# Attention: where the older head's output is turned, who copies and divides it, and two casts on GpSimd

## The chip, the core and the metric

The kernel runs on one core of one Trainium2 chip. The metric is the device time of one execution in microseconds (us). The core's engines work in parallel and each takes its own instructions strictly in the order in which they are written: TensorE (PE) does the matrix products, VectorE (DVE) and ScalarE (ACT) read and write both SBUF and PSUM here, GpSimd (POOL) works on SBUF, and SyncE (SP) starts most of the transfers. They wait for one another through semaphores.

## What is computed

Attention over 16 heads with queries averaged in pairs, a mixture of 8 experts of which each token takes two, and a last two-layer block. Only the first is touched by the change:

```
q_pool = q.reshape(B, H, S // 2, 2, D).mean(axis=3)         # B=2, H=8, S=1152, D=64
scores = scale * np.matmul(q_pool, k.transpose(0, 1, 3, 2)) # 576 x 1152 per head
scores = scores - np.max(scores, axis=-1, keepdims=True)
attn = np.exp(scores)
attn = attn / (np.sum(attn, axis=-1, keepdims=True) + 1e-09)
x = np.matmul(attn, v)                                      # 576 x 64 per head
logits = x @ w_gate                                         # top 2 of 8 experts per token
```

The inputs are float32, and the kernel keeps that accuracy by splitting operands into a high and a low half.

## The kernel before

**Cycles and heads.** The 16 heads pass through a pipeline of 16 cycles, `cycle(p, hh)` on each engine, of which cycle c = 2p + hh does three things at once. It computes the scores and the products with the values of head c - 1 (numbered from 0, so cycle 1 is head 0), prepares head c (keys and queries transposed, 15 trial score blocks "m" from which the row maxima come), and from cycle 2 on it finishes head c - 2: its output lies as columns in `ot`, is turned back to rows by TensorE (`turn_o`, L1475, which also multiplies with the gate weights), and is divided by the row sums. Cycles 3 to 14 are a hardware loop on PE, ACT and DVE. Cycle 15 prepares the last head, and cycle 16 has no head to prepare and instead computes the routing of the first batch on DVE.

**Steps.** A cycle has 9 steps, one for each block of 128 keys; the text numbers them 1 to 9 (`j` + 1 in the code). In a step PE does the four score matmuls (L1490, L1491) and six value matmuls of an earlier step (L1506 to L1508), ACT takes the exponential twice (`ph` at L788, then in place at L793), and DVE subtracts to get the low half (`low_p`, L1035). PE may start the scores of a step only when the low half of the step two before is done, and the products only when their own low half is done.

**Slots and banks.** Around these, `PLACES` puts up to four smaller jobs in each step: "m" a block for the maximum (PE L1460, reduced by DVE at L1023), "n", "k" and the tail transposes of keys and queries (L1446 to L1451), "q" transposes of the queries' low half with the maxima (L1468), and "o" the turn. They share two PSUM banks in turn (`bank_of`), so a job waits until the one two places before it in the list has been emptied (`bank_free`). Before the change "o" is the last job of step 9, followed by ("k", 3) of the next cycle, four transposes, and then by the scores of step 1. Those scores wait for `qb_ev`, ScalarE's copy of the last "q" piece (L740).

**The output's path before.** After `turn_o`, DVE in `o_out` adds 1e-9 to the five row sums (L1046), takes their reciprocals (L1049), and multiplies 320 output columns (L1061) and 80 gate columns (L1062) out of PSUM. The last of these posts `o_norm`.

**GpSimd** splits the keys, queries and values of the coming head into halves (`split_kq`, `split_v`), copies the keys (`copy_k`), and in its last four heads also splits a quarter of the first expert's weights each (`split_weights`). Heads 2 to 11 are a hardware loop.

**The end of attention.** In cycle 16 PE does one turn ("o" in step 9, head 14), then the products of the last two key blocks, then the turn of head 15, and first-tile and rank products that wait for DVE's routing steps.

## Time and profile before

| | |
|---|---|
| three runs | 854.05, 856.22, 857.81 us (median 856.22) |
| the profiled execution | 854.54 us, of which the trace spans 852.8 us |
| PE busy | 838.9 us, 98% of the span |
| DVE, ACT, POOL busy | 499.0, 422.2, 402.5 us (59%, 50%, 47%) |
| granted TensorE clock | 1.00 over the whole span |

The profile is of one execution. A row of a timeline gives start, duration, engine, line, operation, what is written and read, and how many like it were merged; in brackets stands the idle time ahead of it and who ended it. Matmuls overlap in the pipeline: the duration of one is longer than the distance to the next, so a small stall shows only as a greater distance between two starts, and "busy" hides it. A turn is five matmuls in the program and ten in the trace. Attention ends at about 308 us; the rest of the span is experts and the last block.

### The profile page before, as it was taken

Reading aid. Unit: us, or ns where it says so; the run is one execution under the profiler, and the core shown is the slowest. Engines: PE = TensorE matmul, PEld = TensorE weight load, DVE = VectorE, ACT = ScalarE, POOL = GpSimd, SP = SyncE. Lnnn points to the kernel's source line nnn. Section 1 sums busy time; section 2 is a strip of 40 time slices with the busy share of each in tenths; the row PEclk is TensorE's granted clock in tenths of the full one; section 3 lists DMA queues with packets and bytes.
Section 4 is the critical chain, followed back from the end, with each engine's and each line's share of the span. In section 5 each row is a group of like instructions: output and inputs, shape, how many; then the busy total and the mean of one; then the engine's idle time right before and its main releaser. Section 6 shows DMA issues by size and latency. Waiting matters only on the chain.

```text
span 852.8 us, 15404 instructions
## 1 busy us (share of the span) xinstructions
PE 838.9 (98%) x4868; PEld 744.4 (87%) x4869; DVE 499.0 (59%) x995; ACT 422.2 (50%) x776; POOL 402.5 (47%) x293
## 2 busy tenths in 40 slices
PE   7999999999999999999999999999999999999998
PEld 6899999999999888888887888888888888999997
DVE  7788877888877887322232222222276776676664
ACT  3777777777777763212111211111145665564554
POOL 8554445555877104648959959577532030000000
PEclk9999999999999999999999999999999999999999
DMA  5112211142232015987645545363444020000101
GB/s 146 53 43 62 64 42 42 42 142 67 92 130 102 1 56 181 310 298 241 237 151 172 197 148 184 118 214 115 155 133 152 1 75 27 12 1 0 38 1 38
DMA packets 51521, 91.28 MB, mean 107 GB/s; under 512 B 9376, under 2 KB 18592, under 8 KB 50976
## 3 DMA queue, kind: packets, MB, share of 16 engines
q1 hardware_dynamic: 40832, 67.26, 23.5%
q0 software_dynamic: 3360, 11.01, 4.4%
q10 hardware_dynamic: 7296, 12.59, 4.4%
q8 instruction: 19, 0.31, 0.2%
q14 instruction: 14, 0.11, 0.0%
HBM read 73.78 MB, written 17.06 MB: 107 GB/s over the span
## 4 chain that ended last, share of the span: by engine, by line
PE 89%; DVE 5%; ACT 2%; issue 2%; POOL 2%; DMA 0%; DVEq 0%; POOLq 0%; ACTq 0%
PE ps L1640 10%; PE ps L1642 10%; PE ps L1641 10%; PE ps L1460 5%; PE ps L1490 5%; PE ps L1506 4%; PE ps L1508 4%; PE ps L1507 4%; PE ps L1491 4%; PE ps L1766 4%; PE ps L1767 4%; PE ps L1765 4%; PE ps L1752 3%; PE ps L1750 3%; PE ps L1751 3%; PE ps L1679 2%
## 5 line engine op out<-in xcount | busy, mean ns | idle before, releaser
L639 POOL TENSOR_TENSOR W<-stage,W 128x2048 fp32r<-128x2048 f32 x32 | 147.3, 4602 | 2.6
L1023 DVE TENSOR_REDUCE mx<-ps 128x1 f32<-128x384 f32 x225 | 119.6, 551 | 17.8 <-PE ps L1460 17.8
L1035 DVE TENSOR_TENSOR pl__80<-ps,ph 128x576 fp32r<-128x576 f32 x144 | 108.0, 750 | 33.5 <-ACT ps L793 33.4
L788 ACT ACTIVATE ph<-ps 128x576 fp32r<-128x576 f32 x144 | 93.9, 652 | 53.5 <-PE ps L1491 52.4
L793 ACT ACTIVATE ps<-ps 128x576 f32<-128x576 f32 x144 | 93.5, 649 | 0.0
L1506 PE MATMUL ps<-ph,vs 128*65 128x288 f32 x288 | 86.1, 299 | 0.4 <-ACT ot L747 0.4
L862 ACT CAST hh<-ps 128x512 fp32r<-128x512 f32 x50 | 26.9, 590 | 119.2 <-PE ps L1679 115.2
L1490 PE MATMUL ps<-qat,kt 128*128 128x288 f32 x288 | 83.8, 306 | 1.3 <-ACT qbt L740 0.6
L1508 PE MATMUL ps<-ph,vs 128*65 128x288 f32 x288 | 84.8, 294 | 0.0
L1507 PE MATMUL ps<-pl__80,vs 128*65 128x288 f32 x288 | 84.6, 294 | 0.0
L1640 PE MATMUL ps<-W,xh 128*128 (+1 forms) x200 | 80.4, 402 | 1.3 <-POOL W L639 0.7
L1640 PE MATMUL ps<-W,hh 128*128 (+1 forms) x200 | 80.4, 402 | 0.0
L1491 PE MATMUL ps<-qbt,k 128*128 128x288 f32 x288 | 80.3, 294 | 0.0
L1642 PE MATMUL ps<-W,xl 128*128 (+1 forms) x200 | 78.3, 392 | 0.0
L1642 PE MATMUL ps<-W,hl 128*128 (+1 forms) x200 | 78.3, 391 | 0.0
L1641 PE MATMUL ps<-W,hh 128*128 (+1 forms) x200 | 77.9, 390 | 0.0
L1641 PE MATMUL ps<-W,xh 128*128 (+1 forms) x200 | 77.8, 389 | 0.0
L1460 PE MATMUL ps<-kt,qat 128*128 128x384 f32 x225 | 76.2, 352 | 1.6 <-ACT qat L727 0.9
L1300 DVE COPY ys<-ps 128x512 f32<-128x512 f32 x25 | 17.3, 691 | 96.5 <-PE ps L1642 96.5
L1288 DVE TENSOR_SCALAR hid<-ps 128x512 f32<-128x512 f32 x25 | 17.3, 692 | 91.9 <-PE ps L1642 87.7
L1750 PE MATMUL ps<-fh,W 128*128 128x384 f32 x192 | 64.9, 338 | 0.0
L1752 PE MATMUL ps<-fh,W 128*128 128x384 f32 x192 | 64.8, 337 | 0.0
(220 smaller groups left out, 1960.8 us busy)
## 6 DMA issues: line engine op xcount, KB each, us to landing
stage<-in_moe_w_dram SPq DMA_DIRECT2D x32, 1024.0 KB
y_slots<-ys ACTq DMA_DIRECT2D x25, 256.0 KB
x_slots<-ring SPq DMA_DIRECT2D x22, 256.0 KB
xs<-x_slots ACTq DMA_DIRECT2D x22, 256.0 KB
kn<-in_k_dram SPq DMA_DIRECT2D x16, 288.0 KB, 3.3
vn<-in_v_dram SPq DMA_DIRECT2D x16, 288.0 KB, 2.8
stage<-in_moe_w_in_dram SPq DMA_DIRECT2D x4, 1024.0 KB
stage<-in_moe_w_out_dram SPq DMA_DIRECT2D x4, 1024.0 KB
```

The source lines that it names most:

```text
L639: pl.tensor_tensor(W[:, slot, 1, part], stage[:, j % 2, :], W[:, slot, 0, part].bitcast(F32), ALU.subtract).then_inc(w_ready, 1)
L1023: ve.tensor_reduce(mx3[:, i:i + 1], ps[:, bank_of(hh, ("m", i)), 0:PIECE], AX_X, ALU.max).then_inc(m_ev, 1)
L1035: ve.tensor_tensor(pl_[:, j % 3, :].rearrange("p (a n) -> p a n", a=2), ps[:, 2 * s_par(hh, j):2 * s_par(hh, j) + 2, 0:HQ], ph[:, j % 3, : ...
L1460: pe.matmul(ps[:, bank_of(hh, ("m", i)), 0:PIECE], qat[:, par, c * P:(c + 1) * P], kt[:, par, a * PIECE:(a + 1) * PIECE], start=True, stop ...
L1490: pe.matmul(ps[:, 2 * sp_ + a, 0:HQ], kt[:, par, keys], qat[:, par, cols], start=True, stop=False)
L1491: last = pe.matmul(ps[:, 2 * sp_ + a, 0:HQ], k1[:, par, keys], qbt[:, par, cols], start=False, stop=True)
L1506: pe.matmul(dst, vs[:, par, j, 0, :], ph[:, j % 3, cols], start=(j == 0), stop=False)
L1507: pe.matmul(dst, vs[:, par, j, 0, :], pl_[:, j % 3, cols], start=False, stop=False)
L1508: last = pe.matmul(dst, vs[:, par, j, 1, :], ph[:, j % 3, cols], start=False, stop=(j == KC - 1))
L1640: pe.matmul(dst, hi, rhs_of(i, 0), start=(i == 0), stop=False)
L1641: pe.matmul(dst, hi, rhs_of(i, 1), start=False, stop=False)
L1642: last = pe.matmul(dst, lo, rhs_of(i, 0), start=False, stop=(i == n - 1))
```

## The change

"o" moves from the end of step 9 to the end of step 5, behind ("m", 8). In cycles 2 to 15 the turned output is copied as it is from PSUM to a new SBUF tile `raw` by ScalarE (`turned_move`, 405 columns, behind the second exponential of step 5), which posts `o_ev`; DVE computes only the sums and reciprocals, out of `raw`, in step 6 behind its low half (`denominators`); and GpSimd does the two multiplications (`norm`) at the end of its next piece of work. The job that follows in the same bank, ("m", 10), waits for `o_ev` and no longer for `o_norm`. In cycle 16 and for head 15 DVE still does the whole of `o_out`, in cycle 16 now in step 5. DVE's subtraction for step 9, which the old slot "o" carried along, gets a line of its own in the same place. GpSimd's hardware loop over heads 2 to 11 is written out. Its high half of the queries is a cast of `qp` (before: a second addition of both query parts) and waits for `qp`; its high half of the values is a cast (before: an addition of zero).

```diff
-          [("m", 7), ("m", 8)], [("m", 9), ("m", 10)], [("m", 11), ("m", 12)], [("m", 13), ("m", 14), ("n", 0)],
-          [("n", 1), ("q", 0), ("q", 1), ("o", 0)]]
+          [("m", 7), ("m", 8), ("o", 0)], [("m", 9), ("m", 10)], [("m", 11), ("m", 12)],
+          [("m", 13), ("m", 14), ("n", 0)], [("n", 1), ("q", 0), ("q", 1)]]
...
-                pl.tensor_tensor(qa[:, :, :, :].bitcast(F32R), q0.unsqueeze(2).to_broadcast([P, QC, 2, D]),
-                                 q1.unsqueeze(2).to_broadcast([P, QC, 2, D]), ALU.add).then_inc(qa_done, 1)
+                pool.wait_ge(qp_done, m + 1)
+                pl.tensor_copy(qa[:, :, :, :].bitcast(F32R), qp[:, :, :].unsqueeze(2).to_broadcast([P, QC, 2, D])
+                               ).then_inc(qa_done, 1)
...
-                pl.tensor_tensor(vs[:, par, :, 0, 0:D], vn[:, par, :, :],
-                                 zcol[:, :].unsqueeze(2).to_broadcast([P, KC, D]), ALU.add).then_inc(vh_done, 1)
+                pl.tensor_copy(vs[:, par, :, 0, 0:D], vn[:, par, :, :]).then_inc(vh_done, 1)
...
+            def norm(g):
+
+                pool.wait_ge(rinv_done, g + 1)
+                pl.tensor_tensor(x[:, :, g * D:(g + 1) * D], raw[:, :, 0:D],
+                                 rinv[:, :].unsqueeze(2).to_broadcast([P, QC, D]), ALU.mult)
+                pl.tensor_tensor(shares[:, g, :, :], raw[:, :, D + 1:TURN],
+                                 rinv[:, :].unsqueeze(2).to_broadcast([P, QC, 2 * E]), ALU.mult).then_inc(o_norm, 1)
...
+            for m in range(2, NHEAD):
+                split_kq(m // 2, m % 2)
+                copy_k(m - 1, (m - 1) % 2)
+                split_v((m - 1) // 2, (m - 1) % 2)
+                if m > 2:
+                    norm(m - 3)
...
+            def turned_move(p, hh):
+
+                g = 2 * p + hh
+                act.wait_ge(ot_done, g + 1)
+                at_least(act, o_norm, g)
+                sc.copy(raw[:, :, :], ps[:, bank_of(hh, ("o", 0)), 0:QC * TURN].rearrange("p (c d) -> p c d", c=QC)
+                        ).then_inc(o_ev, 1)
...
+            def denominators(p, hh):
+
+                g = 2 * p + hh
+                dve.wait_ge(o_ev, g + 1)
+                at_least(dve, rinv_done, g)
+                ve.tensor_scalar(den_o[:, :], raw[:, :, D], 1e-9, None, ALU.add).then_inc(den_done, 1)
+                at_least(dve, o_norm, g)
+                dve.wait_ge(den_done, g + 1)
+                ve.reciprocal(rinv[:, :], den_o[:, :]).then_inc(rinv_done, 1)
...
-                        if kind == "o" and main:
-                            low_p(p, hh, KC - 1)
-                        if kind == "o" and before:
+                        if kind == "o" and before and not prep:
                             o_out(p, hh - 2)
                         if n == 0 and j > 0 and main:
                             low_p(p, hh, j - 1)
+                        if n == 0 and j == 5 and before and prep:
+                            denominators(p, hh - 2)
+                    if j == KC - 1 and main:
+                        low_p(p, hh, KC - 1)
...
                 elif kind == "o":
-                    at_least(pe, o_norm, h - 1)
+                    at_least(pe, o_ev, h - 1)
```

The order of the instructions shows it in three places. First PE at the border of two cycles. Here L1468 (L1498 after) is the last "q" piece, whose copy by ScalarE the scores wait for, L1475 the turn, L1451 (L1481 after) the four transposes of ("k", 3), and L1490 (L1520 after) the first score matmul. Before:

```order
L1468 MATMUL ps<-ident,qb 128x128
L117 REGISTER_ALU
L1475 ISA
L1475 MATMUL ps<-turner,ot 128x81 x5
L117 REGISTER_ALU x2
L1451 MATMUL ps<-ident,qa 128x128 x4
L1485 REGISTER_ALU
L117 ISA
L1490 MATMUL ps<-qat,kt 128x288
```

After:

```order
L1498 MATMUL ps<-ident,qb 128x128
L117 REGISTER_ALU
L1481 MATMUL ps<-ident,qa 128x128 x4
L1515 REGISTER_ALU
L117 ISA
L1520 MATMUL ps<-qat,kt 128x288
```

The turn has left the stretch between the last "q" piece and the scores that need its copy.

Second PE and DVE at the start of step 6. On PE after the change, L1538 is the last value matmul of step 5, L1505 the turn, and the two L1490 are ("m", 9) and ("m", 10):

```order
L1538 MATMUL ps<-ph,vs 65x288
L117 REGISTER_ALU
L1505 ISA
L1505 MATMUL ps<-turner,ot 128x81 x5
L117 REGISTER_ALU
L1490 MATMUL ps<-kt,qat 128x384
L117 REGISTER_ALU
L1520 MATMUL ps<-qat,kt 128x288
L1521 MATMUL ps<-qbt,k_94 128x288
L1520 MATMUL ps<-qat,kt 128x288
L1521 MATMUL ps<-qbt,k_94 128x288
L1490 MATMUL ps<-kt,qat 128x384
```

On DVE in the same place, L1041 before and behind are the reductions of ("m", 9) and ("m", 10), and L1053 is the low half of step 5:

```order
L1041 TENSOR_REDUCE mx_64<-ps 128x1
L1052 REGISTER_ALU
L1053 TENSOR_TENSOR pl__80<-ps,ph 128x576
L117 REGISTER_ALU
L1063 TENSOR_SCALAR den_o<-raw 128x5
L1066 RECIPROCAL rinv<-den_o 128x5
L1038 REGISTER_ALU
L1041 TENSOR_REDUCE mx_64<-ps 128x1
```

Before the change, PE goes from the value matmuls of step 5 straight to ("m", 9), and DVE from the low half straight to the reduction of ("m", 10).

Third DVE in steps 5 and 6 of cycle 16, where L1035 (L1053 after) are the low halves of steps 4 and 5 and the rows from L1102 (L1130 after) mark which experts a token has. Before:

```order
L1035 TENSOR_TENSOR pl__80<-ps,ph 128x576
L1102 CAST topf<-topi 128x5x2
L1103 MEMSET topf 64x2
L1105 TENSOR_TENSOR onehot<-topf,iota_e 128x8x5 x2
L1108 TENSOR_TENSOR member<-onehot 128x8x5
L1035 TENSOR_TENSOR pl__80<-ps,ph 128x576
```

After:

```order
L1053 TENSOR_TENSOR pl__80<-ps,ph 128x576
L1074 TENSOR_SCALAR den_o<-ps 128x5
L1077 RECIPROCAL rinv<-den_o 128x5
L1089 TENSOR_TENSOR x<-ps,rinv 128x5x64
L1090 TENSOR_TENSOR shares<-ps,rinv 128x80
L1130 CAST topf<-topi 128x5x2
L1131 MEMSET topf 64x2
L1133 TENSOR_TENSOR onehot<-topf,iota_e 128x8x5 x2
L1136 TENSOR_TENSOR member<-onehot 128x8x5
L1053 TENSOR_TENSOR pl__80<-ps,ph 128x576
```

The four operations of `o_out` for head 14 now stand between the two low halves; before they stood behind the last low half of the cycle.

## Rows read from the trace of the kernel before

**Rows 1.** Cycle 10: sum, busy PE, PEld, DVE, ACT, POOL; clock, DMA share, GB/s

```profile
164.31:182.57 18.26, 18.23 (x138) 17.41 (x136) 14.57 (x30) 13.99 (x26) 8.92 (x9) 1.00 0.43 144
```

**Rows 2.** Timeline (start, us, engine line op), border of cycles 9 and 10

```profile
162.86 1.25 PE L1475 MATMUL ps<-turner,ot 65*128 x10
163.08 0.28 ACT L740 CAST qbt<-ps 128x128 fp32r<-128x128 f32 x1
...
163.95 0.60 PE L1451 MATMUL ps<-ident,qa 128*128 128x128 f32 x4
164.31 0.38 PE L1490 MATMUL ps<-qat,kt 128*128 128x288 f32 x1
```

**Rows 3.** Timeline, border of cycles 1 and 2, where no turn stands

```profile
35.09 0.27 PE L1468 MATMUL ps<-ident,qb 128*128 128x128 f32 x1
35.43 0.28 ACT L740 CAST qbt<-ps 128x128 fp32r<-128x128 f32 x1
...
35.81 0.37 PE L1490 MATMUL ps<-qat,kt 128*128 128x288 f32 x1 [0.44 <-issue]
```

**Rows 4.** Timeline, the first "m" jobs of cycle 10, then of cycle 2

```profile
165.70 0.52 PE L1460 MATMUL ps<-kt,qat 128*128 128x384 f32 x2
...
166.17 1.02 DVE L1023 TENSOR_REDUCE mx<-ps 128x1 f32<-128x384 f32 x2 [0.78 <-PE ps L1460]
...
166.78 0.44 PE L1460 MATMUL ps<-kt,qat 128*128 128x384 f32 x1
...
37.79 0.61 PE L1460 MATMUL ps<-kt,qat 128*128 128x384 f32 x2
...
38.88 0.44 PE L1460 MATMUL ps<-kt,qat 128*128 128x384 f32 x1
```

**Rows 5.** Timeline of DVE, sums and reciprocals, then steps 6 and 7

```profile
164.15 0.17 DVE L1046 TENSOR_SCALAR den_o<-ps 128x5 f32<-128x5 f32 x1 [0.19 <-PE ps L1475]
...
164.42 0.19 DVE L1049 RECIPROCAL rinv<-den_o 128x5 f32<-128x5 f32 x1
...
172.91 1.09 DVE L1023 TENSOR_REDUCE mx<-ps 128x1 f32<-128x384 f32 x2
173.91 0.75 DVE L1035 TENSOR_TENSOR pl__80<-ps,ph 128x576 fp32r<-128x576 f32 x1
174.57 1.10 DVE L1023 TENSOR_REDUCE mx<-ps 128x1 f32<-128x384 f32 x2
```

**Rows 6.** Timeline of PE, ("m", 9), ("m", 10) and ("m", 12) of cycle 10

```profile
173.06 0.34 PE L1460 MATMUL ps<-kt,qat 128*128 128x384 f32 x1
...
173.77 0.34 PE L1460 MATMUL ps<-kt,qat 128*128 128x384 f32 x1
...
175.44 0.34 PE L1460 MATMUL ps<-kt,qat 128*128 128x384 f32 x1
```

**Rows 7.** Groups by line and shape, 80 to 220 us: busy, mean ns, idle before

```profile
L747 ACT COPY ot<-ps 65x576 f32<-65x576 f32 x7 | 4.5, 637 | 0.3
L607 POOL TENSOR_TENSOR qp<-qn 128x320 f32<-128x320 f32 x8 | 7.0, 874 | 65.5 <-PE ps L1451 65.5
```

**Rows 8.** Timeline of cycle 16, steps 5 to 7, then its end

```profile
298.93 0.29 PE L1508 MATMUL ps<-ph,vs 128*65 128x288 f32 x1
...
299.12 0.17 DVE L1102 CAST topf<-topi 128x10 f32<-128x10 uint32 x1
...
300.03 0.76 DVE L1035 TENSOR_TENSOR pl__80<-ps,ph 128x576 fp32r<-128x576 f32 x1
...
300.84 0.40 PE L1490 MATMUL ps<-qat,kt 128*128 128x288 f32 x1
...
306.66 0.15 DVE L1046 TENSOR_SCALAR den_o<-ps 128x5 f32<-128x5 f32 x1
...
307.22 0.29 PE L1506 MATMUL ps<-ph,vs 128*65 128x288 f32 x1
...
307.70 0.16 DVE L1117 SCALAR_TENSOR_TENSOR mine<-rank,member 128x5 f32<-128x5 f32 x1
```

More of the change, by code:

```diff
@@ L157, in build @@
         ot_done = sem("ot_done")
+        o_ev = sem("o_ev")
         den_done = sem("den_done")
@@ L321, in build @@
         lg, at = place("lg", at, [P, RT, 2 * E])
+        raw, at = place("raw", at, [P, QC, TURN])
         assert at <= REGION + REGION_BYTES
@@ L613, in split_kq @@
                                  ).then_inc(kl_done, 1)
-                pool.wait_ge(qp_done, m + 1)
                 pool.wait_ge(qa_done, m + 2)
@@ L656, in _ @@
             split_v(0, 0)
-            with pool.Fori(1, NHEAD // 2 - 2) as p:
-                for par in range(2):
-                    split_kq(p, par)
-                    copy_k(2 * p + par - 1, 1 - par)
-                    split_v(p - 1 + par, 1 - par)
-            for m in range(NHEAD - 4, NHEAD):
-                j, par = m - NHEAD + 4, m % 2
-                split_kq(m // 2, par)
-                copy_k(m - 1, 1 - par)
-                split_v((m - 1) // 2, 1 - par)
-                split_weights(0, j, 0, 16 * (j // 2 + 1))
+            for m in range(2, NHEAD):
[4 more added lines that the diff above has]
+                    norm(m - 3)
+                if m >= NHEAD - 4:
+                    j = m - NHEAD + 4
+                    split_weights(0, j, 0, 16 * (j // 2 + 1))
             copy_k(NHEAD - 1, 1)
             split_v(NHEAD // 2 - 1, 1)
+            norm(NHEAD - 3)
             def gather(t, dst, done):
@@ L776, in moves @@
                                 kq_move(p, hh, slot, bank_of(hh, slot))
+                            if prep and before and kind == "o":
+                                turned_move(p, hh - 2)
                             if prep and kind == "q":
```

## The prediction

> **What bounds the kernel now.** Read the busy shares of one cycle first [rows 1]: PE is busy for 18.23 of 18.26 us, DVE for 14.57, ACT for 13.99, GpSimd for 8.92, at a granted clock of 1.00. So PE sets the time, and work taken from DVE is worth nothing unless DVE holds PE up. Busy time can't show that, since matmuls overlap; the starts in the timeline can. Read the border of two cycles [rows 2]: the turn takes PE 1.09 us (162.86 to 163.95), ("k", 3) 0.36, and the scores start at 164.31. During the turn ScalarE makes the copy that these scores wait for, from 163.08 to 163.36. Then the first "m" jobs [rows 4]: ("m", 0) starts at 165.70, DVE reduces it from 166.17, and ("m", 2), which needs its bank, starts at 166.78, 1.08 us behind it. With 0.17 for ("m", 1) and the 0.71 from one "m" to the next over four score matmuls [rows 6] it was due at 166.58: a stall of 0.20 us, and 0.10 more because the first matmul after a stall takes 0.44 instead of 0.34 [rows 4, 6]. But DVE had been idle for 0.78 us when the block came, so the divisions did not cause it. Last DVE in steps 6 and 7 [rows 5]: two reductions and a low half take 1.66 us (172.91 to 174.57) without a gap, and a PE step is as long. DVE has nothing to spare there, and it is there that the change adds to it.
>
> **The border of two cycles.** The 1.09 us of the turn are moved, not saved. PE reaches ("k", 3) at what was 162.86, is done with it at 163.22 and wants to start the scores. ScalarE's chain in step 9 is untouched, so the copy L740 still ends at 163.36. From the end of that copy to the score matmul rows 3 give 0.10 us (35.71 to 35.81), in the one border of the trace that has no turn. The scores start at 163.46: **+0.24 us**. The border without a turn tells the same in another way: 0.72 us lie between the "q" piece and the scores [rows 3]; less the piece's own 0.11 and the 0.36 of ("k", 3), which there comes later, 0.25 are left. Bounds: nothing, if ScalarE gets to L740 earlier, and 0.6, if ("k", 3) covers nothing because it waits itself.
>
> **The turn in step 6.** I count from the end of step 5's value matmuls, 173.06 [rows 6]. The turn runs to 1.09, then ("m", 9) starts. Its reduction starts 0.47 later [rows 4], at 1.56, takes 0.46 to the next start, the low half 0.66 (to 2.68), the sums 0.27 to the start of the reciprocal [rows 5], and that 0.14 (between nothing and its 0.19). So the reduction of ("m", 10) starts at about 3.10 and ends 0.55 later; 0.06 more and ("m", 12) may start: 3.71. By PE's own pace it is due at 1.09 + 2.38 = 3.47 [rows 6]. That is a stall of 0.24, and the restart costs 0.10, as at ("m", 2): **+0.34 us**. Between 0.08 (only PE's change from narrow to wide matmuls) and 0.60. The idle us of DVE during the turn doesn't help, because the low half of step 5 is queued behind the reduction of ("m", 9).
>
> From there DVE runs one step behind where it was, and has no slack to catch up: ("m", 14) is reduced about 0.09 later relative to PE, the second key transposes wait for that bank, and ScalarE's chain of step 9 starts from them: **+0.09 us** (0 to 0.2).
>
> ScalarE's copy of 405 columns is in no row. Copies of 128 and 576 columns take 0.28 and 0.64 [rows 2, 7], so about 0.50 lies between. The turn's end reaches its reader 1.29 us after its start (162.86 to 164.15) [rows 2, 5]. The copy ends at 1.79 and ("m", 10), which waits for it, may start at 1.89; it is due at 1.09 + 0.71 = 1.80 and 0.1 for the change of width. **Nothing**, up to 0.2 if the copy is longer. ScalarE waits for the turn, with the exponentials of step 6 queued behind, but their scores are not ready before about 2.0.
>
> **GpSimd.** The multiplication of 320 columns costs about what L607 costs, 0.87 [rows 7], that of 80 less; say 1.2 together, and the two casts give about as much back. Ahead of L607 GpSimd is idle for 65.5 us in 8 cycles [rows 7], 8.2 each, and the next user of `x` is a head later. Cost nothing, as long as that idle time is there. In the four last heads the weights take most of it; then GpSimd starts its next head some tenths late, with results due many us later. The hardware loop that is written out falls under the same cover. The Trainium skill (GPSIMD Engine Reference, 4.1 Engine selection) speaks against the move: elementwise work of two inputs belongs on VectorE, GpSimd being about two times slower. The trace agrees: of the 1.04 us that DVE needs for all of `o_out` [rows 8] the two multiplications are 0.63, against my 1.2. But under that idle time the sum is the same by either price.
>
> So one cycle costs 0.24 + 0.34 + 0.09 = 0.67 us. Cycles 2 to 14 are **13 x 0.67 = 8.7 us**. Cycle 15 has no ("k", 3) behind it and DVE is fuller there: the turn's 1.09 is added, the scores of cycle 16 come 0.36 earlier behind their copy than now, and about 0.2 of DVE waits is added: **+0.9 us**.
>
> **Cycle 16.** DVE's `o_out` for head 14 goes in front of the marking of experts and the low half of step 5 [rows 8]. PE ends step 5's products at 299.06 (the last starts at 298.93, and 0.13 lie between two). The turn's result is there 1.29 later, 300.35; `o_out` takes 1.04 (306.66 to 307.70), the marking 0.91 (299.12 to 300.03), so the low half starts at 302.30 instead of 300.03, 2.27 later. The scores of step 7 wait for it and shift as much, to 303.1, while PE is through with the turn and the 1.33 us of step 6 at about 301.5 and idles for 1.6. At the end the turn of step 9 is gone. The last low half is now done at about 306.8 (`o_out` starts right behind it, at 306.66); 2.27 later, at 309.1, the last products can start, and now they start at 307.22: **+1.9 us** (1.2, if only the turn's 1.04 counted back, to 2.3). The routing that follows needs this end, so it shows in full.
>
> **Sum.** 8.7 + 0.9 + 1.9 = 11.5 us. On the profiled execution's 854.54 that is 866.0; this execution lies 1.7 below the median of the runs shown, on which it would be 867.7. I forecast **867 us**.
>
> **Rivals.** (1) *The stalls of "m" go, and it is faster.* If moving the divisions let DVE take ("m", 0) earlier, the 0.30 us at ("m", 2) would go, and at most as much at ("m", 4) and ("m", 5), the other place where two blocks stand back to back: 13 x 0.6 = 7.8 us, 847 to 848, if no new wait comes. It decides if a block's bank comes back in 0.88 us instead of 1.08. Against it: in cycle 2 no division stands ahead, and the distance is 1.09 us all the same (37.79 to 38.88) [rows 4]. Chance 0.07.
> (2) *DVE's two small operations are hidden.* Then only the border, the change of width and the end are left: 13 x 0.32 + 0.4 + 1.9 = 6.5, about 861 to 862. Chance 0.15.
> (3) *Nearly all is hidden*, because ScalarE's chain shifts with PE and the end of attention has slack: 0 to 4 us, 855 to 860. For it: every wait found is a few tenths. Chance 0.15.
> (4) *The bank of the turn comes back late*, ScalarE's copy taking 0.3 longer than between its neighbours: 13 x 0.3 = 4 more, 871. Chance 0.07.
> (5) *The clock falls* in the new pause of cycle 16. At 1.2 in place of 2.4 GHz the 8 us of matmuls behind it (300.84 to 309) would take 16: about 874. The granted clock is 1.00 over the whole span, also behind the 0.44 us of idle PE at 35.8 [rows 3]; a pause of 1.6 is in no row. Chance 0.04. In the Trainium skill (TensorE: Matmul & The Clock Gate, HAM oscillation) pauses of PE bring its clock down; this trace shows none that did.
> The forecast keeps 0.52.
>
> The range of 8 in 10 goes from 859.5 (most of rival 3 left out) to 871.5. A measurement of this kernel can tell about 0.5% from no change, 852 to 860.5: faster 0.06, same 0.16, slower 0.78.
>
> **What would show it.** In the profile after: the score matmul behind ("k", 3) starts 0.10 us after L748's copy, with 0.6 us between it and ("k", 3)'s first transpose; a cycle is 18.9 to 19.0 us instead of 18.26; ("m", 12) starts 2.7 us after ("m", 9) instead of 2.38; ("m", 10) doesn't wait; in cycle 16 PE pauses ahead of step 7. I am wrong if a cycle is still 18.3 us (DVE was not full, or ScalarE earlier than I think), or shorter.

## The result and the profile after

| | before | after |
|---|---|---|
| median, us | 855.51 (854.05 to 857.81, 4 runs) | 864.94 (863.91 to 865.74, 4 runs) |
| ratio | | 1.0114, 95% interval 1.0099 to 1.0129 |
| profiled execution: time, span | 854.54, 852.8 | 865.51, 863.8 |

The change makes the kernel 1.1% slower: 9.4 us by the medians. The prediction had said 867.

One word on counting. What the prediction and the rows ahead of it call cycle 10 (from 164.31 us) is the ninth cycle if the one from 17.68 us is the first, and the border in front of it is that of cycles 8 and 9. From here on cycles are counted so, from the first score matmul of each. Nothing else hangs on it. Where each stage begins gives the bill, in us:

| stage | before | after | difference |
|---|---|---|---|
| cycle 1 | 18.13 | 20.02 | +1.89 |
| cycle 2 | 18.82 | 19.40 | +0.58 |
| cycles 3 to 14, each | 18.271 | 18.818 | +0.55, in all 6.57 |
| cycle 15 | 17.70 | 18.38 | +0.68 |
| cycle 16, to the last value products | 16.30 | 18.22 | +1.92 |
| from there to the first expert matmul | 18.38 | 18.40 | +0.02 |

This makes 11.7; what follows attention is 0.7 shorter in this execution, for a reason that wasn't looked for, and the spans differ by 11.0.

The profile's line of busy time, then one cycle of after in the busy shares (columns as in [rows 1]):

```profile
PE 846.8 (98%) x4868; PEld 748.0 (87%) x4869; DVE 487.5 (56%) x967; ACT 428.2 (50%) x790; POOL 395.7 (46%) x321
...
151.18:170.00 18.82, 18.75 (x135) 17.51 (x135) 13.80 (x28) 14.42 (x29) 8.63 (x11) 1.00 0.15 47
```

DVE has 11.5 us less to do than before, 0.77 less in a cycle [rows 1], and the cycle is 0.55 longer. PE shows as busy for 18.75 of 18.82: the lost time is again in no gap, only between starts. The border is the first place (timeline; it answers to [rows 2, 3]):

```profile
169.37 0.60 PE L1481 MATMUL ps<-ident,qa 128*128 128x128 f32 x4
169.59 0.28 ACT L748 CAST qbt<-ps 128x128 fp32r<-128x128 f32 x1
...
170.00 0.40 PE L1520 MATMUL ps<-qat,kt 128*128 128x288 f32 x1
```

("k", 3) takes 0.36, but 0.63 us lie between its first transpose and the scores. They start 0.13 behind the end of ScalarE's copy (169.87), which in before ended under the turn. Step 6 is the second place:

```profile
159.96 1.24 PE L1505 MATMUL ps<-turner,ot 65*128 x10
161.00 0.42 PE L1490 MATMUL ps<-kt,qat 128*128 128x384 f32 x1
161.24 0.50 ACT L763 COPY raw<-ps 128x405 f32<-128x405 f32 x1 [0.85 <-PE ps L1505]
...
161.46 0.56 DVE L1041 TENSOR_REDUCE mx<-ps 128x1 f32<-128x384 f32 x1 [1.11 <-PE ps L1490]
...
161.79 0.45 PE L1490 MATMUL ps<-kt,qat 128*128 128x384 f32 x1
161.93 0.75 DVE L1053 TENSOR_TENSOR pl__80<-ps,ph 128x576 fp32r<-128x576 f32 x1
...
162.60 0.16 DVE L1063 TENSOR_SCALAR den_o<-raw 128x5 f32<-128x5 f32 x1
...
162.86 0.19 DVE L1066 RECIPROCAL rinv<-den_o 128x5 f32<-128x5 f32 x1
...
162.97 1.02 DVE L1041 TENSOR_REDUCE mx<-ps 128x1 f32<-128x384 f32 x2
...
163.58 0.45 PE L1490 MATMUL ps<-kt,qat 128*128 128x384 f32 x1
```

("m", 9), ("m", 10) and ("m", 12) start at 161.00, 161.79 and 163.58. The last two show 0.45, the mark of a first matmul after a stall: ("m", 10) came just as ScalarE's copy let its bank go (161.74), ("m", 12) just as DVE was through with ("m", 10). Neither is late by more than a hundredth or so, and each restart costs 0.11. From ("m", 9) to ("m", 12) it is 2.58, against 2.38 in [rows 6]; from the turn's start to the matmul behind ("m", 12) it is 1.35 more than before, and 1.09 of that is the turn: step 6 loses 0.26. Start to start it is made of four terms: 0.08 behind ("m", 9), which follows the turn's narrow matmuls (0.26 in place of 0.18 to the next; the prediction calls this the change of width), 0.11 behind ("m", 10) and 0.11 behind ("m", 12), less 0.04 that the turn itself is shorter here than at the border. And the stall at ("m", 2) is what it was, with DVE idle for 1.40 ahead of it instead of 0.78 [rows 4]:

```profile
152.59 0.51 PE L1490 MATMUL ps<-kt,qat 128*128 128x384 f32 x2
153.05 1.02 DVE L1041 TENSOR_REDUCE mx<-ps 128x1 f32<-128x384 f32 x2 [1.40 <-PE ps L1490]
...
153.66 0.44 PE L1490 MATMUL ps<-kt,qat 128*128 128x384 f32 x1
```

1.07 us from ("m", 0) to ("m", 2): the divisions had never held it. In cycle 16 the low half of step 5 waits behind `o_out` (it answers to [rows 8]), and the last products come as much later:

```profile
312.01 0.76 DVE L1053 TENSOR_TENSOR pl__80<-ps,ph 128x576 fp32r<-128x576 f32 x1
...
312.82 0.40 PE L1520 MATMUL ps<-qat,kt 128*128 128x288 f32 x1 [1.43 <-DVE pl__80 L1053]
...
318.84 0.34 PE L1536 MATMUL ps<-ph,vs 128*65 128x288 f32 x1 [0.35 <-DVE pl__80 L1053]
```

Cycle 1 was in no step of the prediction. Here it costs 1.89 us, of two kinds. One is the new order of banks. In the list the turn stands between ("m", 8) and ("m", 9), so in a cycle without a turn these two follow each other in one bank, half a step apart:

```profile
28.38 0.29 PE L1538 MATMUL ps<-ph,vs 128*65 128x288 f32 x1
28.97 0.45 PE L1490 MATMUL ps<-kt,qat 128*128 128x384 f32 x1 [0.29 <-DVE mx L1041]
```

The same two in before:

```profile
27.03 0.29 PE L1508 MATMUL ps<-ph,vs 128*65 128x288 f32 x1
27.16 0.34 PE L1460 MATMUL ps<-kt,qat 128*128 128x384 f32 x1
```

That is 0.59 in place of 0.13, and 0.11 for the restart: 0.57. The other 1.3 us are the clock in this execution. From 22.0 to 25.5 us TensorE ran at 1.2 GHz, two score matmuls 0.24 apart instead of 0.13 (the granted clock is the first number behind the brackets):

```profile
22.00:26.00 4.00, 3.96 (x17) 3.81 (x18) 3.27 (x6) 1.40 (x3) 3.78 (x6) 0.57 0.02 5
```

Before has 1.00 in this stretch. Three of the kernels below (e1, e3 and f3) have the new place, too, and a granted clock of 1.00 here; their cycle 1 is 18.68 to 18.71, which is the 0.57 alone; and e4, which has the old place, ran at 1.2 GHz from 20.8 to 24.2. Two of the four runs of after, this one among them, show a mean clock of 0.998 and are 1.5 us longer than the two with 1.000; runs of before show such a mean too. Without it the spans differ by 9.7, near the 9.4 of the medians.

### The profile page after: what moved, and what is told of

Its sections match the earlier page's. It is cut to its first block, busy times and chain, and to the rows that moved or that the text cites. A ratio compares the mean times of both kernels' runs of the same rounds, so it can differ in the third digit from the quotient of the medians.

```text
span 863.8 us, 15344 instructions
## 1 busy us (share of the span) xinstructions
PE 846.8 (98%) x4868; PEld 748.0 (87%) x4869; DVE 487.5 (56%) x967; ACT 428.2 (50%) x790; POOL 395.7 (46%) x321
## 4 chain that ended last, share of the span: by engine, by line
PE 87%; DVE 6%; ACT 2%; DMA 2%; POOL 2%; issue 1%; DVEq 0%; POOLq 0%; ACTq 0%
PE ps L1670 10%; PE ps L1672 10%; PE ps L1671 9%; PE ps L1490 6%; PE ps L1520 5%; PE ps L1536 4%; PE ps L1538 4%; PE ps L1537 4%; PE ps L1521 4%; PE ps L1796 3%; PE ps L1797 3%; PE ps L1795 3%; PE ps L1782 3%; PE ps L1780 3%; PE ps L1781 3%; PE ps L1481 2%
## 5 line engine op out<-in xcount | busy, mean ns | idle before, releaser
L1041 DVE TENSOR_REDUCE mx<-ps 128x1 f32<-128x384 f32 x225 | 118.0, 550 | 43.2 <-PE ps L1490 43.1
L1053 DVE TENSOR_TENSOR pl__80<-ps,ph 128x576 fp32r<-128x576 f32 x144 | 108.0, 750 | 34.5 <-ACT ps L811 34.4
L1520 PE MATMUL ps<-qat,kt 128*128 128x288 f32 x288 | 84.3, 308 | 3.6 <-DVE pl__80 L1053 1.7
L1538 PE MATMUL ps<-ph,vs 128*65 128x288 f32 x288 | 85.2, 296 | 0.0
L1490 PE MATMUL ps<-kt,qat 128*128 128x384 f32 x225 | 80.3, 372 | 2.0 <-ACT qat L735 0.9
```

The costliest lines, as they stand in the source:

```text
L1041: ve.tensor_reduce(mx3[:, i:i + 1], ps[:, bank_of(hh, ("m", i)), 0:PIECE], AX_X, ALU.max).then_inc(m_ev, 1)
L1053: ve.tensor_tensor(pl_[:, j % 3, :].rearrange("p (a n) -> p a n", a=2), ps[:, 2 * s_par(hh, j):2 * s_par(hh, j) + 2, 0:HQ], ph[:, j % 3, : ...
L1490: pe.matmul(ps[:, bank_of(hh, ("m", i)), 0:PIECE], qat[:, par, c * P:(c + 1) * P], kt[:, par, a * PIECE:(a + 1) * PIECE], start=True, stop ...
L1520: pe.matmul(ps[:, 2 * sp_ + a, 0:HQ], kt[:, par, keys], qat[:, par, cols], start=True, stop=False)
L1538: last = pe.matmul(dst, vs[:, par, j, 1, :], ph[:, j % 3, cols], start=False, stop=(j == KC - 1))
```

## Experiments

Times are medians; each ratio is to runs of before on the same chip. "Cycle" is the mean of cycles 3 to 14 of the profiled execution, the last two columns are its cycles 15 and 16; all in us. Edits are shown in part; "..." marks what is left out. In e4, f3 and all g kernels except g1 GpSimd divides one head later than in after.

| kernel | time | ratio, 95% interval | cycle | 15 | 16 |
|---|---|---|---|---|---|
| before | 855.0 to 856.2 | | 18.271 | 17.70 | 16.30 |
| after | 864.94 | 1.0114 (1.0099 to 1.0129) | 18.818 | 18.38 | 18.22 |
| e1_last_turn_late | 863.45 | 1.0089 (1.0060 to 1.0119) | 18.803 | 18.37 | 16.27 |
| e2_casts_only | 854.54 | 0.9996 (0.9977 to 1.0015) | 18.271 | 17.71 | 16.27 |
| e3_place_only | 874.27 | 1.0216 (1.0177 to 1.0255) | 19.477 | 19.14 | 18.22 |
| e4_engines_only | 856.09 | 1.0011 (0.9992 to 1.0030) | 18.294 | 17.72 | 16.29 |
| f5_late_wait | 860.77 | 1.0055 (1.0033 to 1.0077) | 18.524 | 17.64 | 18.49 |
| f2_late_wait_before | 854.21 | 0.9982 (0.9967 to 0.9996) | 18.256 | 17.71 | 16.33 |
| f3_divisors_late | 864.46 | 1.0109 (1.0076 to 1.0142) | 18.693 | 18.03 | 18.27 |
| g1_reordered | 864.11 | 1.0092 (1.0068 to 1.0116) | 18.971 | 18.07 | 16.60 |
| g3_m0_early | 852.23 | 0.9968 (0.9957 to 0.9978) | 18.115 | 17.42 | 16.27 |
| g2_after_mended | 854.84 | 1.0000 (0.9988 to 1.0011) | 18.302 | 17.11 | 16.59 |
| g5_gpsimd_waits | 850.61 | 0.9925 (0.9908 to 0.9942) | 17.949 | 17.43 | 16.35 |
| g4_sums_from_psum | 853.27 | 0.9964 (0.9951 to 0.9977) | 18.127 | 17.55 | 16.32 |

**The change taken apart.** e1 is after with the turn of cycle 16, and DVE's `o_out` for it, back in step 9:

```diff
+LAST = [[slot for slot in step if slot != ("o", 0)] for step in PLACES]
+LAST[-1].append(("o", 0))
-                    for n, slot in enumerate(PLACES[j]):
+                    for n, slot in enumerate((PLACES if prep else LAST)[j]):
```

> The changed kernel with one part undone: in cycle 16 the turn of head 14, and DVE's o_out for it, stand in step 9 again. Theory (three places pay: the cycle's border, step 6, and cycle 16's routing queue): the pause of 1.6 us ahead of step 7's scores goes, and the run is 1.9 us under the changed kernel, about 863.0 with it at 864.9. Rival (the routing that follows attention has slack, so a pause in cycle 16 costs nothing): no difference, 864.9.

Cycle 16 is 16.27 us again, 1.95 less; the median is 1.5 less, where 1.9 was expected. e2 is before with the two casts and GpSimd's loop written out:

```diff
-                pl.tensor_tensor(qa[:, :, :, :].bitcast(F32R), q0.unsqueeze(2).to_broadcast([P, QC, 2, D]),
-                                 q1.unsqueeze(2).to_broadcast([P, QC, 2, D]), ALU.add).then_inc(qa_done, 1)
+                pool.wait_ge(qp_done, m + 1)
+                pl.tensor_copy(qa[:, :, :, :].bitcast(F32R), qp[:, :, :].unsqueeze(2).to_broadcast([P, QC, 2, D])
+                               ).then_inc(qa_done, 1)
...
-                pl.tensor_tensor(vs[:, par, :, 0, 0:D], vn[:, par, :, :],
-                                 zcol[:, :].unsqueeze(2).to_broadcast([P, KC, D]), ALU.add).then_inc(vh_done, 1)
+                pl.tensor_copy(vs[:, par, :, 0, 0:D], vn[:, par, :, :]).then_inc(vh_done, 1)
```

> The kernel before with only GpSimd's two casts and its loop over heads written out; the turn, the copy and the divisions as before. Theory: GpSimd ends each head 1.3 us earlier, nobody waits for it, 855.5 within 1 us. Rival (the straight code or the casts are part of what the change costs): some of the 9.4 us appears here, 857 or more.

No cycle differs from before by more than 0.04. Each cast is cheaper (0.72 for 1.56, 0.66 for 1.14), under idle time of GpSimd. e3 is before with the new `PLACES` alone, DVE still dividing out of the bank; e4 is after with the old `PLACES`:

```diff
 e3, to before
-          [("m", 7), ("m", 8)], [("m", 9), ("m", 10)], [("m", 11), ("m", 12)], [("m", 13), ("m", 14), ("n", 0)],
-          [("n", 1), ("q", 0), ("q", 1), ("o", 0)]]
+          [("m", 7), ("m", 8), ("o", 0)], [("m", 9), ("m", 10)], [("m", 11), ("m", 12)],
+          [("m", 13), ("m", 14), ("n", 0)], [("n", 1), ("q", 0), ("q", 1)]]
 e4, to after (its PLACES as in before), and
-                if m > 2:
-                    norm(m - 3)
+                if m > 3:
+                    norm(m - 4)
```

> The kernel before with only the turn moved to the end of step 5; DVE does all of o_out there, straight out of PSUM, ahead of the reduction of (m, 9). Theory (the place costs): the border pays 0.28 us as in the changed kernel, and (m, 10) now waits for the whole o_out, 1.29 + 1.04 + 0.1 = 2.4 us after the turn's start against 1.8 due, 0.6 and a restart of 0.1; about 1.0 us in 14 cycles, 0.6 in cycle 1, 1.9 in cycle 16: 872. Rival (the copy by ScalarE and the hand-over to GpSimd cost, the place is free): 858 or less.

> The changed kernel with the turn back at the end of step 9 in every cycle; ScalarE still copies, DVE still makes the reciprocals (behind the last low half), GpSimd still divides (one head later, so that it doesn't wait at the border) and still casts. Theory (the place costs): the turn covers ScalarE's copy at the border again, step 6 is as before, cycle 1 has no stall of 0.59 at (m, 9): 855.5 to 857, since ScalarE's copy now stands between the border's copies and may push (k, 3)'s by a tenth. Rival (copy and hand-over cost): 861 or more.

The place costs 1.21 us a cycle with the old engines and 0.52 with the new ones. e3 came out above its forecast (874.27 against 872, 1.21 a cycle against 1.0), e4 within its own. In e3 ("m", 10) stands 1.54 behind ("m", 9), since the bank comes back only when `o_out` is through:

```profile
163.79 0.42 PE L1460 MATMUL ps<-kt,qat 128*128 128x384 f32 x1
164.04 0.17 DVE L1046 TENSOR_SCALAR den_o<-ps 128x5 f32<-128x5 f32 x1 [0.89 <-PE ps L1475]
...
165.04 0.23 DVE L1062 TENSOR_TENSOR shares<-ps,rinv 128x80 f32 x1
...
165.33 0.44 PE L1460 MATMUL ps<-kt,qat 128*128 128x384 f32 x1 [0.59 <-DVE shares L1062]
```

So the new engines repair more than half of what the new place does, and without it they bring nothing: 18.294. The loss is the place's.

**The border.** The scores of step 1 need the late copy only in their second half of queries. f5 (on after) and f2 (on before) let PE wait for it there:

```diff
                 if j == 0:
                     pe.wait_ge(k1_done, h + 1)
-                    pe.wait_ge(qb_ev, 2 * (h + 1))
+                    pe.wait_ge(qb_ev, 2 * h + 1)
...
                     pe.matmul(ps[:, 2 * sp_ + a, 0:HQ], kt[:, par, keys], qat[:, par, cols], start=True, stop=False)
+                    if j == 0 and a == 1:
+                        pe.wait_ge(qb_ev, 2 * (h + 1))
```

> After, with one wait moved: the scores of step 1 read the query copy of 128 columns (the one that ends last in step 9) only in their fourth matmul, so the wait for it stands in front of that matmul and no longer in front of the first. Theory of the prediction: TensorE stands 0.24 to 0.28 us at every border because this copy ends late and the turn no longer covers it. Three matmuls take 0.39, so the wait must go: a cycle 18.82 -> 18.56 us, 14 borders x 0.26 = 3.6 us, about 861.3 against 864.9 of after. Rival: the border is held by something that stands behind the same time (ScalarE's exponentials or the low halves): a cycle stays 18.8 and the time 864 to 865.

> Before, with the same wait moved in front of the fourth score matmul. Theory: in before the turn of 1.09 us lies beside the copy, so nothing waits there and nothing changes: a cycle stays 18.27 us, the time 855.5 (854.5 to 856). Rival: the wait instruction itself, or a bank behind it, costs something at the border of before too: then a cycle is 0.05 to 0.1 us shorter, 854.

In f5 the scores start 0.36 behind ("k", 3), with the copy still running, and a cycle is 0.29 shorter:

```profile
147.32 0.60 PE L1481 MATMUL ps<-ident,qa 128*128 128x128 f32 x4
147.54 0.28 ACT L748 CAST qbt<-ps 128x128 fp32r<-128x128 f32 x1
...
147.68 0.38 PE L1520 MATMUL ps<-qat,kt 128*128 128x288 f32 x1
```

f2 leaves the cycle as it was (18.256) and helps only where before has no turn, at the first border (cycle 1 is 0.68 shorter, cycle 2 then 0.40 longer). By the medians it is 0.8 us, just clear of noise though the forecast said no change; the first border, which the forecast left out, gives 0.3 of it net. The border's price is shown, and that the turn hid it.

**VectorE in step 6.** f3 puts DVE's sums and reciprocal of after behind the last low half (GpSimd's later division is not shown):

```diff
-                        if n == 0 and j == 5 and before and prep:
-                            denominators(p, hh - 2)
                     if j == KC - 1 and main:
                         low_p(p, hh, KC - 1)
+                    if j == KC - 1 and before and prep:
+                        denominators(p, hh - 2)
```

> After, with VectorE's two small operations (sums and reciprocal, 0.4 us) moved from step 6 to step 9 behind the last low half, where VectorE waits anyway, and GpSimd's multiplications one head later. The turn stays behind step 5. Theory: of the 0.26 us that step 6 loses, these two operations hold ('m', 12) (its restart 0.10 and a few hundredths), the rest is the turn's bank at ('m', 10) and the change of width: a cycle 18.82 -> 18.71 us, 13 x 0.11 = 1.4 us, about 863.4. Rival A: all of the loss of step 6 comes through VectorE: 18.56, about 861.5. Rival B: the low half of step 5 and the two reductions are late by themselves, the small operations cost nothing: 18.82, 864.9.

18.693, 0.125 less, and ("m", 12) stands unstalled 1.77 behind ("m", 10). The theory's number was 18.71. But the median gave only 0.5 of the 1.5 us back: its four runs lie between 863.2 and 867.7, and the profiled one starts attention 0.4 late. In it the clock also fell to 1.2 GHz from 334.9 to 338.3, behind attention, where the profiled execution of after has 1.00; what follows attention is 2.0 longer than in after. The cycle decides here, not the median. ("m", 10) keeps its restart.

**A better order, first try.** g1 changes the list more: with the turn between ("m", 9) and ("m", 10), ("k", 3) a cycle early, and ("m", 0) ahead of the products. The late wait, cycle 16's turn in step 9 and the code that carries ("k", 3) over are not shown:

```diff
+PLACES = [[None, ("m", 0)], [("m", 1), ("m", 2)], [("m", 3), ("m", 4)], [("m", 5), ("m", 6)],
+          [("m", 7), ("m", 8), ("m", 9)], [("o", 0), ("m", 10)], [("m", 11), ("m", 12)],
+          [("m", 13), ("m", 14), ("n", 0)], [("n", 1), ("q", 0), ("q", 1), ("k", 3)]]
```

> After, with the list written anew: the turn at the head of step 6, a step behind ('m', 8) in its bank and with ('m', 9) ahead of it, ('m', 11) next in its bank; the next head's last query transposes ('k', 3) at the end of step 9 instead of the start of step 1; ('m', 0) between scores and products of step 1, so that no 'm' stands less than 1.1 us behind the one with its bank; the late wait of the scores in front of their fourth matmul; cycle 16's turn in step 9 as before. Theory: every stall of a cycle found so far is gone: the 0.26 of the border, the 0.26 of step 6 less about 0.05 for the change of width, and also the 0.30 at ('m', 2) that before has too. A cycle is 17.95 to 18.05 us instead of 18.27 (before) and 18.82 (after), cycle 16 as before: 855.1 - 13 x 0.27 = 851.6, 850.5 to 852.5, the first of these kernels ahead of before. Rival: VectorE or ScalarE gives out elsewhere when TensorE runs closer (a new wait for an exponential in step 1, behind the copy of 512 columns that now stands in front of it): a cycle of 18.2 to 18.3, 854 to 856.

It failed: 18.97 us. I had taken away two waits and made two:

```profile
151.45 0.63 ACT L737 CAST qat<-ps 128x512 fp32r<-128x512 f32 x1
...
152.14 0.44 PE L1489 MATMUL ps<-kt,qat 128*128 128x384 f32 x1 [0.24 <-ACT qat L737]
...
159.95 1.09 DVE L1042 TENSOR_REDUCE mx<-ps 128x1 f32<-128x384 f32 x2
...
160.64 1.34 PE L1504 MATMUL ps<-turner,ot 65*128 x10 [0.20 <-DVE mx L1042]
```

("m", 0) reads what ("k", 3)'s copy writes, and this copy is last in ScalarE's queue; and a block of a step's second place is reduced behind the low half, so that its bank comes back 1.50 us after its start (159.14), not 1.08. I had used one round trip for all. With their restarts the two waits cost 0.36 to 0.51 and about 0.42 us a cycle, most of the 0.97 by which the cycle is over its forecast.

**Second try.** g3 is e4 with three edits, g2 the same on after (with e1's and f3's edits). The blocks read the query columns in another order, ("m", 0) the last 128, whose copy is done in step 9:

```diff
-PLACES = [[("k", 3), None, ("m", 0)], ...
+PLACES = [[("k", 3), ("m", 0)], ...
-                if i == 0:
-                    pe.wait_ge(kq_ev, 4 * (h + 1))
+                if i < 2:
+                    pe.wait_ge(kq_ev, 4 * h + 3 + i)
                 a, c = divmod(i, QC)
+                c = (c - 1) % QC
```

and f5's late wait.

> The change's division of work (ScalarE copies, GpSimd divides, casts) with the turn back in step 9, and three edits: ('m', 0) between scores and products of step 1; the 15 'm' blocks in another order of query columns, so that ('m', 0) reads the columns whose copy is done in step 9 and ('m', 1) the first that needs ('k', 3); the late wait of the scores. The turn's bank is the one ('m', 0) uses next: ScalarE's copy gives it back about 0.6 us after the turn, VectorE's whole o_out would need 1.2 and would be late. Theory: the 0.30 us of every cycle at ('m', 2), which before has too, comes only from ('m', 0), ('m', 1) and ('m', 2) standing within 0.88 us where a bank needs 1.08. With 1.66 between them it is gone and nothing else changes: a cycle 18.29 -> 17.99 us, 14 x 0.3 = 4.2 us, 851.5 against 855.0 to 856.1. Rival: VectorE or ScalarE makes another matmul wait at once, since all three run closer: a cycle of 18.2 or more, 854 to 855.5.

> After with all that was found undone where it can be: the turn stays behind step 5 (cycle 16's in step 9), the late wait of the scores, VectorE's sums and reciprocal behind the last low half, and ('m', 0) early with the other order of columns, as in the run beside this. Theory, from terms measured one at a time: 18.82 - 0.29 (border) - 0.13 (sums and reciprocal) - 0.30 (at ('m', 2)) = 18.10 us a cycle, 0.1 more than the run beside this one, because the turn costs a restart at ('m', 10) and a change of width; the time 852.5 to 853.5. Rival: the terms don't add up, since each wait that goes lets the next come late (the sums and reciprocal now stand where VectorE's low half of step 9 must be early): 18.3 or more, 855 to 857.

g3 is faster than before by 0.3%, with 0.18 us a cycle of the 0.30 that it should have gained: from cycle 5 on its cycles alternate between about 18.35 and 17.95 us. g2 only gets back to before: 18.30 a cycle and 854.84, where the theory had 18.10 and 852.5 to 853.5; the rival's cycle of 18.3 came true. It is 0.19 behind g3, not 0.1. The missing part of g3 is in DVE's sum over five columns:

```profile
162.41 0.88 POOL L609 TENSOR_TENSOR qp<-qn 128x320 f32<-128x320 f32 x1 [9.14 <-PE ps L1481]
162.45 0.86 DVE L1065 TENSOR_SCALAR den_o<-raw 128x5 f32<-128x5 f32 x1 [0.72 <-ACT raw L764]
162.69 0.34 PE L1491 MATMUL ps<-kt,qat 128*128 128x384 f32 x1
...
163.41 0.19 DVE L1068 RECIPROCAL rinv<-den_o 128x5 f32<-128x5 f32 x1
...
164.01 1.02 DVE L1043 TENSOR_REDUCE mx<-ps 128x1 f32<-128x384 f32 x2 [0.41 <-PE ps L1491]
...
164.62 0.44 PE L1491 MATMUL ps<-kt,qat 128*128 128x384 f32 x1
```

0.86 us for what takes 0.16 in after. It ends at 163.31, 0.02 behind the end of GpSimd's L609. ("m", 0), started at 162.69, is reduced only from 164.01, and ("m", 2) stalls at 164.62. In the next cycle the sum takes 0.77, but the reduction follows the reciprocal at once (181.93), and nothing stalls. Here 0.41 us lie between the two, and so it is in the first cycle of every pass but the first of VectorE's hardware loop, whose body is two cycles; the profile names no work there. It takes both, the long sum and this gap, to make the stall. g2 has the same two, and the same stall in the same cycles (about 18.46 against 18.18):

```profile
164.17 0.88 POOL L611 TENSOR_TENSOR qp<-qn 128x320 f32<-128x320 f32 x1 [9.39 <-PE ps L1483]
...
165.78 1.02 DVE L1045 TENSOR_REDUCE mx<-ps 128x1 f32<-128x384 f32 x2 [0.41 <-issue]
...
166.39 0.44 PE L1493 MATMUL ps<-kt,qat 128*128 128x384 f32 x1
```

Its other cycles are 0.24 behind g3's: 0.08 more behind ("m", 0), 0.08 for the change of width, 0.11 for the restart at ("m", 10), less 0.04 for the shorter turn. g2 with g5's wait below was not run.

**The two engines.** g5 is g3 with one wait more on GpSimd; g4 takes the sums from the bank instead, ahead of ScalarE's copy (the waits of PE and GpSimd that this needs are not shown):

```diff
 g5, to g3 (split_kq)
+                at_least(pool, rinv_done, m - 3)
 g4, to g3 (denominators, turned_move)
-                dve.wait_ge(o_ev, g + 1)
-                ve.tensor_scalar(den_o[:, :], raw[:, :, D], 1e-9, None, ALU.add)
+                dve.wait_ge(ot_done, g + 1)
+                ve.tensor_scalar(den_o[:, :], turned[:, :, D], 1e-9, None, ALU.add)
+                act.wait_ge(den_done, g + 1)
```

> The kernel of the m0-early run with one wait more: GpSimd's first sum of a head (320 columns, 0.88 us) waits for VectorE's reciprocal. In the m0-early run VectorE's sum over 5 columns (den_o from raw) takes 0.77 or 0.86 us where it takes 0.16 in after; each time it ends 0.02 to 0.03 us behind the end of the GpSimd instruction that started just before or after it, and ('m', 0) is then reduced late, so that ('m', 2) waits 0.3 in every cycle and 0.4 in every second. Theory: two engines reach for the same way into SBUF and the second stands until the first is through. With GpSimd behind it the sum takes 0.17 again, ('m', 0) is reduced 0.47 behind its start, and a cycle is 17.9 to 17.95 us in place of 18.115 (mean): 12 to 13 times 0.2 = 2.5 us, 849.7 against 852.2. GpSimd starts 0.4 later with 9 us idle in hand. Rival: the sum is slow because ScalarE's copy of ('k', 3) or the profile's start time makes it look so: it stays at 0.8 and the time at 852.

> The kernel of the m0-early run, but VectorE takes the sums from the turn's PSUM bank, before ScalarE copies it (the copy waits for that), and not from the copy in SBUF. Theory as in the run beside this: the sum starts about 161.9 instead of 162.45 in the cycle that starts at 162.08, takes 0.17, and both small operations are through when GpSimd starts; ScalarE's copy is 0.2 later and ends at 162.65, just as ('m', 0) is due: a cycle of 17.95 to 18.05 us, 849.7 to 851. Rival: ScalarE's later copy pushes ('k', 3)'s copy and the exponentials, and a cycle stays at 18.1: 852.

g5, the border of the same cycle:

```profile
163.79 0.17 DVE L1066 TENSOR_SCALAR den_o<-raw 128x5 f32<-128x5 f32 x1 [0.71 <-ACT raw L765]
...
164.03 0.34 PE L1492 MATMUL ps<-kt,qat 128*128 128x384 f32 x1
164.07 0.19 DVE L1069 RECIPROCAL rinv<-den_o 128x5 f32<-128x5 f32 x1
164.57 0.88 POOL L610 TENSOR_TENSOR qp<-qn 128x320 f32<-128x320 f32 x1 [9.04 <-DVE rinv L1069]
...
165.70 0.33 PE L1492 MATMUL ps<-kt,qat 128*128 128x384 f32 x1
```

The sum takes 0.17, the gap of 0.41 behind the reciprocal is still there, ("m", 2) starts at 165.70 without a stall, and every cycle is 17.95. **850.61 against 856.21 us: 0.75% faster than before** (interval 0.6 to 0.9%), the fastest kernel here, with the change's division of work and not its place. Its forecast was 849.7. Cycles 3 to 14 give 3.9 us of the gain and cycle 1 (16.98 in place of 18.13) 1.15. Its profiled execution starts attention at 19.78 instead of 17.68, as e1's and g1's do about; why was not looked into. That GpSimd and ScalarE must share the division for it is argued, not shown: no run has these edits on before, with DVE dividing. g4's sum takes 0.16 too, but ScalarE's copy starts 0.2 later (162.54) and ends at 163.04, where ("m", 0) waits for the bank and restarts (0.44 at 163.10): 18.13 a cycle. Its theory's upper end was 18.05: it had the bank free "just as" it was due, and that is again a restart. The rival had it right with 18.1, and the median of 853.27 is above both.

## Why the prediction was right, and where not

- **What bounds the kernel, and rival 1.** Right: ("m", 0) to ("m", 2) is 1.07 us in after with DVE idle for 1.40 ahead of it. DVE's share fell and nothing was gained.
- **The border, +0.24.** Right, 0.03 low: 0.63 less 0.36 is 0.27, since 0.13 us, not 0.10, lie between the copy's end and the scores. f5 gets 0.29 back, f2 next to nothing in a cycle.
- **Step 6, +0.34.** The mechanism was right (low half, sums and reciprocal in front of the reduction that ("m", 12) waits for), the size was off: 0.26. Counted from the turn's start, the reduction of ("m", 10) began at 3.01, where I had 3.10, and ("m", 12) was due at 3.61, where I had 3.47, the restart of ("m", 10) and the change of width being in it. So the stall of 0.24 shrank to a tie with its restart of 0.11; f3 takes 0.125 away.
- **("m", 10) doesn't wait, 0.** Wrong by a restart. The copy's 0.50 was right (499 ns in the profile), but it ended at 1.78 after the turn's start, and the block started at 1.83 with 0.45. I had it due at 1.90 and free at 1.89: a tie, in which the cost is not the hundredths but the 0.1 of the restart. This is most of what f3 left.
- **DVE's lag of 0.09.** Wrong: nothing. The border's 0.29 (f5) and step 6's 0.26 are the whole 0.55 of a cycle, and between step 6 and the border no distance between two starts is more than 0.02 longer than before.
- **A cycle, 0.67.** It was 0.55: 7.15 in place of 8.7 us for cycles 2 to 14. Here lies most of the 2 us by which the forecast was high. The signs named for it say the same: a cycle was to be 18.9 to 19.0 and is 18.82, ("m", 12) was to start 2.7 behind ("m", 9) and starts 2.58 behind. Rival 2 (DVE's operations hidden, 861 to 862) had too little: f3 shows them at work.
- **Cycle 15, +0.9.** It was 0.68; the 0.2 for waits of DVE was not there. **Cycle 16, +1.9.** It was 1.92, and 1.95 by e1; PE's pause in it was 1.43, not 1.6.
- **GpSimd and the casts, 0.** Right in after and e2. The price of the two multiplications was 1.05 (0.73 and 0.32), not 1.2, and 1.6 times VectorE's 0.64. But the cover I named, idle time, is not all that counts there. I had not asked what GpSimd does to VectorE; in after the sums stand in step 6, where GpSimd is idle, so the question didn't arise.
- **Missing: cycle 1.** I followed the list only through cycles that have all kinds of slot. Without a turn ("m", 8) and ("m", 9) share a bank: 0.57 us. That the forecast lies within 2.1 us is in part luck: 1.8 us too much in cycles 2 to 15 stand against this 0.57 that was left out.

## What to carry to other kernels

Work that looks like a cost on the critical engine may be the cover of a wait: before moving it, ask what ends beneath it (here ScalarE's copy, 0.29 us a cycle). Of a ring of banks, follow every occupant to the next one, in each kind of cycle and at each place of the queue that frees it: 0.88 us between two users of a bank that takes 1.08 cost 0.3, and the place in the queue made it 1.50. Each of the three ties met here, ("m", 10) and ("m", 12) in after and ("m", 0) in g4, cost a full restart, so count one for a predicted tie; and a small operation on an idle engine can still be held by another engine.

## What the runs showed of the hardware

**VectorE's small operation from SBUF to SBUF stands while GpSimd's instruction runs.** `den_o<-raw` took 0.16 with GpSimd idle (after), and 0.85, 0.56 and 0.86 in e4, f3 and g3 (0.57 in g2), each time to 0.02 or 0.03 us behind the end of GpSimd's `qp<-qn`, whether it started 0.04 or 0.34 behind it:

```profile
165.83 0.87 POOL L609 TENSOR_TENSOR qp<-qn 128x320 f32<-128x320 f32 x1 [9.45 <-PE ps L1480]
165.88 0.85 DVE L1064 TENSOR_SCALAR den_o<-raw 128x5 f32<-128x5 f32 x1 [0.71 <-ACT raw L764]
...
168.42 0.87 POOL L609 TENSOR_TENSOR qp<-qn 128x320 f32<-128x320 f32 x1 [9.93 <-PE ps L1482]
168.76 0.56 DVE L1064 TENSOR_SCALAR den_o<-raw 128x5 f32<-128x5 f32 x1
```

(e4, then f3.) The reciprocal beside GpSimd's cast was not held (0.19 at 163.41 in g3), nor were low halves, which read one side from PSUM (0.75 at 182.87 in g3). The Trainium skill (SBUF — State Buffer, Who interferes with whom) says that the two engines share a pair of SBUF ports as an exclusive lock, held for a whole instruction, and that a tensor_scalar can take it. The trace agrees: the second stood, and was not merely slower. In e4 it went with about 0.08 us in every second cycle (18.34 against 18.26) and no more, because ("m", 2) stalled anyway; only with that stall gone did it show in full. Whether the sum from PSUM would run beside GpSimd wasn't seen: in g4 it was through before GpSimd began.

**A restart costs 0.10 to 0.11 us however short the stall**: 0.44 or 0.45 instead of 0.34 for a 384-column matmul, also where it waited for hundredths (161.79 in after).

**The clock fell in some executions and not in others**: to a mean of 0.57 between 22 and 26 us in after, where before has 1.00, though TensorE had been busy for the same 4.11 of the 6 us ahead of it in both. What decides it is not settled. It also fell to 1.2 GHz once behind attention in the profiled executions of e3, e4, f3, f5 and g1 (334.9 to 338.3 in f3), and not in those of before and after. In cycle 16's pause of 1.4 us in after, where rival 5 had feared it, the clock stayed at 1.00.
